# Fused attention and two-layer MLP: the next pair's main scores in one stretch

## What is computed

```
scores = q @ k.T / 8, causal mask, softmax over the keys -> a;  local = a @ v
phi(x) = elu(x) + 1;  mem_out = (phi(q) @ M_prev) / (phi(q) . z_prev + 1e-6)
x = g * mem_out + (1 - g) * local,   g = sigmoid(beta) by head
```

## Time and profile before

| | |
|---|---|
| time, median of 3 runs | 1036.76 us (1036.2 to 1037.63) |
| profiled execution, its own time | 1037.46 us |
| profiled execution, span | 1035.7 us |
| PE busy | 1015.5 us (98%) |
| PE weight load busy | 930.8 us (90%) |
| DVE busy | 489.7 us (47%) |
| ACT busy | 412.2 us (40%) |
| POOL busy | 273.9 us (26%) |
| granted PE clock, mean | 0.999 |
| share of PE in the chain that ended last | 96% |

### The profile page before, as it was taken

One profiled execution on the slowest core, in us unless ns is written; L12 is line 12 of the kernel. 1 busy time (PEld: TensorE's weight loads), 2 busy tenths in 40 slices (PEclk: granted clock), 3 DMA queues, 4 the chain that ended last, 5 costly groups with the idle time before them and its releaser, 6 DMA issues.

```text
span 1035.7 us, 16398 instructions
## 1 busy us (share of the span) xinstructions
PE 1015.5 (98%) x6256; PEld 930.8 (90%) x6256; DVE 489.7 (47%) x1063; ACT 412.2 (40%) x935; POOL 273.9 (26%) x276
## 2 busy tenths in 40 slices
PE   5999999999999999999999999999999999999998
PEld 3777777779999999999999999999999999999997
DVE  5888888865544444444444443323223233232222
ACT  4777777753323233232332554223222222232222
POOL 6788888868500000000000465000000000000000
PEclk9999999999999999999999999999999999999999
DMA  5544555413200000000000242000000000000000
GB/s 169 146 143 143 146 141 144 123 44 92 72 1 2 1 0 0 0 0 0 1 1 1 82 133 83 1 1 31 1 30 0 0 30 0 31 1 1 31 1 31
DMA packets 30204, 48.02 MB, mean 46 GB/s; under 512 B 3264, under 2 KB 13504, under 8 KB 30144
## 3 DMA queue, kind: packets, MB, share of 16 engines
q1 hardware_dynamic: 27584, 38.81, 12.5%
q0 software_dynamic: 2560, 8.39, 2.8%
HBM read 42.47 MB, written 4.72 MB: 46 GB/s over the span
## 4 chain that ended last, share of the span: by engine, by line
PE 96%; DVE 1%; DMA 1%; POOL 1%; issue 0%; SPq 0%; ACT 0%; POOLq 0%; DVEq 0%; ACTq 0%
PE ps L904 26%; PE ps L903 26%; PE ps L902 26%; PE ps L869 4%; PE ps L797 4%; PE ps L778 3%; PE ps L857 2%; PE ps L846 2%; PE ps L785 1%; DVE probT L639 1%; PE ps L839 1%; PE ps L822 1%; PE ps L782 1%; DMA qraw<-in_qT 0%; PE ps L832 0%; DMA braw<-in_bN 0%
## 5 line engine op out<-in xcount | busy, mean ns | idle before, releaser
L904 PE MATMUL ps<-xparts,W 128*128 128x384 f32 x768 | 257.8, 336 | 0.0
L902 PE MATMUL ps<-xparts,W 128*128 128x384 f32 x768 | 257.6, 335 | 0.0
L903 PE MATMUL ps<-xparts,W 128*128 128x384 f32 x768 | 257.2, 335 | 0.0
L717 DVE TENSOR_TENSOR glo<-act_t,ghi 128x384 fp32r<-128x384 f32 x192 | 110.8, 577 | 220.7 <-ACT ghi L503 220.7
L503 ACT CAST ghi<-act_t 128x384 fp32r<-128x384 f32 x192 | 98.7, 514 | 229.8 <-PE ps L904 210.8
L300 POOL TENSOR_TENSOR W<-stage,W 128x512 fp32r<-128x512 f32 x64 | 83.0, 1306 | 324.7 <-ACT W L545 321.7
L902 PEld LDWEIGHTS ps<-xparts,W 128*128 128x128 f32 x768 | 144.2, 188 | 4.2
L903 PEld LDWEIGHTS ps<-xparts,W 128*128 128x128 f32 x768 | 144.1, 188 | 4.1
L904 PEld LDWEIGHTS ps<-xparts,W 128*128 128x128 f32 x768 | 144.1, 188 | 0.0
L902 PE MATMUL ps<-ghi,W 128*128 128x384 f32 x384 | 128.3, 334 | 0.0
L904 PE MATMUL ps<-ghi,W 128*128 128x384 f32 x384 | 128.3, 334 | 0.0
(11 more groups left out here) (109 smaller groups left out, 1384.5 us busy)
## 6 DMA issues: line engine op xcount, KB each, us to landing
qraw<-in_qT SPq DMA_DIRECT2D x16, 320.0 KB, 3.5
vn<-in_vN SPq DMA_DIRECT2D x16, 320.0 KB, 3.8
kraw<-in_kT SPq DMA_DIRECT2D x16, 288.0 KB, 2.8
qn<-in_qN SPq DMA_DIRECT2D x16, 288.0 KB, 2.8
zb<-in_zN SPq DMA_DIRECT2D x32, 144.0 KB, 4.1
out_x<-ostage SPq DMA_DIRECT2D x18, 256.0 KB, 2.0
stage<-in_moe_w_in POOLq DMA_DIRECT2D x16, 256.0 KB, 3.7
stage<-in_moe_w_out POOLq DMA_DIRECT2D x16, 256.0 KB, 3.1
```

Source lines behind the costliest of these rows:

```text
L717: nc.vector.tensor_tensor(glo[:, f % SLOTS, :], a, ghi[:, f % SLOTS, :].bitcast(F32), ALU.subtract).then_inc(glo_done, 1)
L902: nc.tensor.matmul(dst, w_lo_, x_hi_, start=first, stop=False)
L903: nc.tensor.matmul(dst, w_hi_, x_lo_, start=False, stop=False)
L904: return nc.tensor.matmul(dst, w_hi_, x_hi_, start=False, stop=last)
```

## The change

Units 0 to 3 of the next pair are issued in one stretch behind T21. S0 and S1 share banks 0 and 1 (columns 0 to 127 and 128 to 383) and one semaphore step; S2 has banks 2 and 3; S3 has banks 6 and 7, those of X. T30, T31 and TAIL follow each other. S4 goes to columns 224 to 799, across banks 0 and 1, as two halves of 288 columns, three matmuls each. New waits: S0 waits for all nine maxima of the pair before, S3 for `x_free`, S4 for maxima 0 to 3, and `memory` for maxima 0 to 7 of the next pair. On DVE the eviction of T1 comes before `to_x`, and the maxima of the next pair are spread around the evictions of T21 and T31. On ACT exponentials 0 and 1 come before the eviction of T30, and PHI's eviction before exponential 4. The host puts the 64 tail keys ahead of the 512 main keys.

```diff
--- before.py
+++ after.py
@@ -115,16 +115,17 @@
             return ps[:, 4 + u % 2, :]
 
 
-        UNITS = FULL + 1
-
-        def score_bank(p, s):
-            return 2 * ((UNITS * p + s) % 2)
-
-
-        READ = [2, 4, 6, 8, 9]
-
-        def reads(unit):
-            return NB * (unit // UNITS) + READ[unit % UNITS]
+
+        UNITS = FULL
+        U_BANK = [0, 2, 6, 0]
+        U_OF = [0, 0, 1, 2, 3]
+        HALF = S // 2
+
+        def score_at(s, e):
+
+            if s == FULL:
+                return BANK * U_BANK[3] + BANK - HALF, S
+            return BANK * (U_BANK[U_OF[s]] + e) + (P if s == 1 else 0), keys(s)
 
 
         TURNS = 10
@@ -459,10 +460,11 @@
                 empty_main(p, T_M20, 2, 0)
                 if more:
                     phi_part_2(p + 1)
-                empty_main(p, T_M30, 3, 0)
                 if more:
                     exps(p + 1, 0)
                     exps(p + 1, 1)
+                empty_main(p, T_M30, 3, 0)
+                if more:
                     exps(p + 1, 2)
                 else:
                     split_x(0, 0, 0)
@@ -474,10 +476,9 @@
                     split_x(0, 0, 2)
                     split_x(0, 0, 3)
                 empty_rest(p)
+                empty_phi(p)
                 if more:
                     exps(p + 1, 4)
-                empty_phi(p)
-                if more:
                     exps(p + 1, 5)
                 empty_row(p)
                 if more:
@@ -580,14 +581,13 @@
 
             def maximum(p, c):
                 m, e = c // 2, c % 2
-                dve.wait_ge(s_full, UNITS * p + m + 1)
-                at = BANK * (score_bank(p, m) + e)
+                dve.wait_ge(s_full, UNITS * p + U_OF[m] + 1)
+                at, n = score_at(m, e)
+                src = flat[:, at:at + n]
                 if m < FULL:
-                    n = keys(m)
-                    src, over = flat[:, at:at + n], mask[:, D + MAIN + P - n:]
-                    dst = prob[:, e, tri(m) * P:tri(m) * P + n]
+                    over, dst = mask[:, D + MAIN + P - n:], prob[:, e, tri(m) * P:tri(m) * P + n]
                 else:
-                    src, over, dst = flat[:, at + BANK - D:at + BANK + MAIN], mask[:, 0:S], ptail[:, D:]
+                    over, dst = mask[:, 0:S], ptail[:, D:]
                 nc.vector.tensor_tensor_reduce(out=dst, in0=src, in1=over, scale=-SCALE, scalar=BIG, op0=ALU.add,
                                                op1=ALU.min, accum_out=negmax[:, p % 2, c:c + 1]).then_inc(s_read, 1)
 
@@ -666,31 +666,33 @@
             dve.wait_ge(made, 12)
             for p in range(NPAIR):
                 more, more2 = p + 1 < NPAIR, p + 2 < NPAIR
+                empty_second(p)
                 if p:
                     to_x(p - 1)
-                empty_second(p)
                 rows(p, 0)
                 rows(p, 1)
+                if more:
+                    maximum(p + 1, 0)
+                    maximum(p + 1, 1)
                 empty_main(p, T_M21, 2, 1)
                 rows(p, 2)
                 rows(p, 3)
                 if more:
-                    for c in range(6):
+                    maximum(p + 1, 2)
+                    maximum(p + 1, 3)
+                empty_main(p, T_M31, 3, 1)
+                if more:
+                    for c in range(4, 8):
                         maximum(p + 1, c)
-                empty_main(p, T_M31, 3, 1)
                 if more2:
                     low_k(p + 2)
                 if more:
-                    maximum(p + 1, 6)
-                    maximum(p + 1, 7)
+                    maximum(p + 1, 8)
                 if more2:
                     low_q(p + 2)
                 if more:
-                    norms(p + 1, 0)
-                    norms(p + 1, 1)
-                    maximum(p + 1, 8)
-                    norms(p + 1, 2)
-                    norms(p + 1, 3)
+                    for step in range(4):
+                        norms(p + 1, step)
             dve.sem_inc(h_free, H_BANKS)
             for k_ in range(KC):
                 split_x(k_, 0, 0, k_)
@@ -763,28 +765,30 @@
         @block.tensor
         def _(pe):
             def score(p, s):
-                g = UNITS * p + s
+                i = p % 2
+                three_of = ((qlo[i], khi[i]), (qhi[i], klo[i]), (qhi[i], khi[i]))
                 if s == 0:
                     pe.wait_ge(lo_done, 2 * p + 2)
-                if g >= 2:
-                    pe.wait_ge(s_read, reads(g - 2))
-                bank = score_bank(p, s)
-                i = p % 2
-                three_of = ((qlo[i], khi[i]), (qhi[i], klo[i]), (qhi[i], khi[i]))
+                    if p:
+                        pe.wait_ge(s_read, NB * p)
+                if s == 3:
+                    pe.wait_ge(x_free, p)
                 if s < FULL:
                     for part, (a, b_) in enumerate(three_of):
                         for e in range(2):
                             r = slice(e * D, e * D + D)
-                            last = nc.tensor.matmul(ps[:, bank + e, 0:keys(s)], a[r, s * P:(s + 1) * P],
-                                                    b_[r, 0:keys(s)], start=(part == 0), stop=(part == 2))
+                            at, n = score_at(s, e)
+                            last = nc.tensor.matmul(flat[:, at:at + n], a[r, s * P:(s + 1) * P], b_[r, D:D + n],
+                                                    start=(part == 0), stop=(part == 2), skip_group_check=True)
                 else:
-                    for part, (a, b_) in enumerate(three_of):
-                        nc.tensor.matmul(ps[:, bank, BANK - D:BANK], a[:, MAIN:], b_[:, MAIN:S],
-                                         start=(part == 0), stop=(part == 2))
-                    for part, (a, b_) in enumerate(three_of):
-                        last = nc.tensor.matmul(ps[:, bank + 1, :], a[:, MAIN:], b_[:, 0:MAIN],
-                                                start=(part == 0), stop=(part == 2))
-                last.then_inc(s_full, 1)
+                    pe.wait_ge(s_read, NB * p + 4)
+                    at, n = score_at(s, 0)
+                    for c0, c1 in ((0, HALF), (HALF, S)):
+                        for part, (a, b_) in enumerate(three_of):
+                            last = nc.tensor.matmul(flat[:, at + c0:at + c1], a[:, MAIN:], b_[:, c0:c1],
+                                                    start=(part == 0), stop=(part == 2))
+                if s:
+                    last.then_inc(s_full, 1)
 
             def room(p, u):
                 if TURNS * p + u >= 2:
@@ -851,6 +855,8 @@
             def memory(p):
                 pe.wait_ge(m_in[p % 2], 16 * (p // 2 + 1))
                 pe.wait_ge(x_free, p + 1)
+                if p + 1 < NPAIR:
+                    pe.wait_ge(s_read, NB * (p + 1) + 8)
                 pe.wait_ge(ev_act, len(BY_ACT) * p + BY_ACT.index(T_PHI) + 1)
                 for c0, c1 in ((0, CUT), (CUT, S)):
                     for e in range(2):
@@ -872,7 +878,7 @@
                 last.then_inc(values_done, 1)
 
             pe.wait_ge(made, 12)
-            for s in range(UNITS):
+            for s in range(FULL + 1):
                 score(0, s)
             for p in range(NPAIR):
                 more = p + 1 < NPAIR
@@ -881,13 +887,10 @@
                 turn_corner(p)
                 turn_one(p, T_M21, 2, 1)
                 if more:
-                    score(p + 1, 0)
-                    score(p + 1, 1)
+                    for s in range(FULL):
+                        score(p + 1, s)
                 turn_one(p, T_M30, 3, 0)
                 turn_one(p, T_M31, 3, 1)
-                if more:
-                    score(p + 1, 2)
-                    score(p + 1, 3)
                 turn_tail(p)
                 if more:
                     score(p + 1, 4)
@@ -982,7 +985,8 @@
     tail = s - main
 
 
-    kt = k.transpose(0, 1, 3, 2).reshape(n, 2 * d, s)
+
+    kt = _np.concatenate([k[:, :, main:], k[:, :, :main]], axis=2).transpose(0, 1, 3, 2).reshape(n, 2 * d, s)
     qt = q.transpose(0, 1, 3, 2).reshape(n, 2, d, s)
     qt2 = _np.zeros((n, 2, d, main + 2 * tail), q.dtype)
     qt2[..., :main] = qt[..., :main]
```

## The result

The changed kernel takes 1031.22 us (median of 5 runs, 1030.98 to 1031.83) against 1036.76 of the kernel before: a ratio of 0.9948, 95% interval 0.9937 to 0.9958.

A forecast was written before the change was run, and what follows sets the result against it. PE was taken as the bound, with only the attention stage open to change. Fourteen pairs at -2.05, pair 0 at -0.3 and the last pair at +0.35 gave -2.0 us: 1036.76 to 1034.7, range 1031.5 to 1037.3.

The forecast's parts named there:

- the stretch: On PE, S0 to S3 issued together: fewer changes between transposes and scores, 0.36 us saved a pair.
- TAIL's new wait: On PE ahead of TAIL: 0.48 us waiting for ACT's eviction of T30, so TAIL starts 0.12 later.
- S4 costs 0.87: On PE, S4 as 288 + 288: forecast 0.88 us instead of 1.14, 0.26 less a pair.
- T21's 0.34: PE's idle time ahead of T21, waiting for DVE's eviction of T1: forecast to stay unchanged at 0.34 us.
- the last pair: Pair without scores beside it: gains nothing, REST comes later through POOL's `weigh`, +0.35 us.
- Rival D: Weight loads not hidden in S4: 1.42 us rather than 0.88, 1043.0 in all; chance 0.11 with any failed cover.
- rival C: Merging scores on PE saves only half of the 0.36 us: 1037.4 in all; chance 0.14.
- the waits and moves that I cost at nothing: Waits and moves across PE, DVE, ACT and POOL, each held to be covered, most by 0.5 to 1.0 us: cost nothing.
- TAIL to S4: On PE, from TAIL's start at 132.47 to S4's at 133.0: no saving counted.
- Pair 0: First pair, partly at half rate: merging about 0, S4's cut -0.26, together -0.3 us.
- the second eviction: On DVE, T1's eviction put ahead of `to_x`: worth 0.01 us, taken as nothing, bounds 0 and 0.04.
- Rival B: At the start, PE reaches and keeps 2.4 GHz in pair 0: 2.5 us less, 1032.2 in all; chance 0.27.

The follow-up runs named there:

- e1: Changed kernel with exponential 4 ahead of PHI's eviction on ACT again: 1033.05 us, ratio to before 0.9962.
- e2: Kernel before with only PHI's eviction moved ahead of exponential 4 on ACT: 1034.91 us, ratio 0.998.
- e4: Kernel before with S4 cut as 288 + 288 in its old banks, tail keys first: 1033.29 us, ratio 0.9965.
- e7: Changed kernel with PE's old order (S0 S1, T30 T31, S2 S3, TAIL, S4) in the new banks: 1040.5 us, ratio 1.0036.
- e10: As e7, but DVE evicts T21 ahead of maxima 0 and 1: 1029.79 us, ratio 0.9933.
- e5: Kernel before with only S4's cut 288 + 288 and PHI's early eviction, old banks and old order on PE and DVE: 1031.41 us, ratio 0.9948.
- e6: Changed kernel with DVE's `to_x` ahead of the eviction of T1 again: 1032.44 us, ratio 0.9954.
- e11: Changed kernel with 20 unread matmuls between S4 and T0 of pair 0, filling PE's pause at the start: 1028.85 us, ratio 0.9926.
- e8: Changed kernel with S4's first half between T31 and TAIL, its second half behind TAIL: 1026.0 us, ratio 0.9895.

## Why the prediction was wrong

**Right.** The direction, and each step that I worked out from a distance: the stretch saves 0.36 (S0 to T30 2.12), TAIL's new wait is 0.48 and puts it 0.12 later, S4 costs 0.87. T21's 0.34 is unchanged, the last pair loses (L639 to the first MLP matmul 10.30 instead of 10.09, so 0.2 and not 0.35). The rule of the Trainium skill (TensorE: Matmul & The Clock Gate, The mechanism) that a load overlaps a matmul only in other row groups is not what happened: 0.13 a matmul (129.41 and the next four starts) is the stream alone. The same section also names a background weight buffer, for which a load is pulled ahead; I had left that out. Rival D is refuted. So is rival C: T30 stands 2.12 behind S0, and with half of the saving gone it would be 2.29. Two slips in rival D changed nothing: at 0.17 a matmul a pair comes out 0.10 worse, not 0.12, and rows with 128 rows of weights and 128 or 192 columns (transposes, values) do exist.

**Wrong, first: "the waits and moves that I cost at nothing".** The move of PHI's eviction stood in my description of the change and has no term in the sum. I had looked only at what the new order could break and not at what the old one held up: L442 had ended 0.12 ahead of `memory`'s first load. It is worth 0.14 us a pair, about 2.0 in all (e1, e2).

**Wrong, second: TAIL to S4 taken as PE's own time.** I took 132.35 to 132.87 over into the changed kernel as 0.52 of work. Without the wait S4's first load comes 0.38 behind TAIL's, so 0.13 of it was the wait for maximum 5; e4 shows the wait with the cut alone, e7 and e10 show 0.38 and 0.39 without it in the same order on PE. At 0.13 a pair it is about 1.8 us. With these two the sum is -2.0 - 2.0 - 1.8 = -5.8, against -5.5. Pair 0 is a smaller miss: I gave it and the start 0.3, and the first L639 of the chain comes 0.9 earlier; half of that (0.46) is there already at pair 0's T21, and its cause was not looked for.

**Wrong in one kernel, right in another: the second eviction.** Where DVE has room it is worth nothing that shows, as I said of the kernel before: e5, which leaves it out, has the changed kernel's time. In the changed kernel it holds off a loop through DVE and PE that is 0.09 a pair longer (e6). The sum had no term for DVE's room at the start of a pair, which went from 0.86 ahead of `to_x` to 0.48 ahead of T1's eviction.

**Rival B** was half right: the clock rose at the start, in S4, as it said, and the pause took it back, as it feared. It had the price right (2.5 us by rows, 2.1 in the time, e11). That the time measured, 1031.22, lies nearer to its 1032.2 than to my 1034.7 is chance: T21 of pair 0 still lasted 0.90, and T21 to TAIL 6.45. The statement of the Trainium skill (same page, What's actually happening) that activity opens the clock and idleness closes it agrees with both traces.

## What to carry to other kernels

An engine that overlaps its operations hides its waits: a wait of 0.1 us leaves no idle row, so compare the start of each step with the end of everything it waits for, before calling a distance work. For every step that a change moves, ask also what the old place held up, not only what the new one may delay. And where two orders on two engines were written for each other, moving one alone can cost more than the whole change brought (e7).

## What was not expected of the hardware

PE fell back to 1.2 GHz in a pause of 4.33 us (changed kernel) and stayed at 2.4 GHz over pauses of 0.49 and 1.55 us (e11). The column of the granted clock can mislead at the start: from 21 to 26 us it reads 1.00 in the kernel before and 0.50 in the changed one, whose trace has a fall in it, and T21 lasts 0.90 in both; from 8 to 13 us it reads 1.00 in both, though the first row of S0 lasts 0.47 against 0.33 later. And S4, of the same tiling as the transposes around it, leaves no idle loads when it is set beside TAIL, and only its first step is longer, 0.22 to 0.24 instead of 0.13 (e8); the 64-row tiling of S0 to S3 leaves loads idle for 0.17 each time it is entered.
